# Weights laid out by partitions, x copied out of PSUM by ScalarE, another order in the tail of local attention, and the second channel weights a stage sooner

## The reference

```python
# 1: local attention, 8 heads of 64: |i - j| < 16 from the tokens themselves,
#    and 24 summaries of 32 tokens each (max of k, mean of v)
k_sum, v_sum = k.reshape(B,H,24,32,D).max(3), v.reshape(B,H,24,32,D).mean(3)
a = softmax([where(|i-j|<16, q k^T/8, -1e9), q k_sum^T/8 + log(32)]);  x = a @ [v; v_sum]
# 2: four experts, each a causal attention of one head of 64, two of four by a gate
logits = x @ w_gate;  w = softmax over the two largest
for e in range(4):
    out += w[e] * (softmax(causal((x @ wq[e]) (x @ wk[e])^T / 8)) @ (x @ wv[e])) @ wo[e]
# 3: mixing over tokens, then over channels
u = x + (relu(x^T @ w_tok1) @ w_tok2)^T
return u + relu(u @ w_ch1) @ w_ch2
```

## Time and profile before

| | us |
|---|---|
| median of 3 runs | 454.16 (452.81 to 454.59) |
| the profiled execution | 454.81 |
| its span, first to last instruction | 453.0 |
| PE busy | 432.1 (95%) |
| DVE busy | 300.1 (66%) |
| ACT busy | 219.9 (49%) |
| POOL busy | 150.6 (33%) |

### The profile page before, as it was taken

One profiled execution on the slowest core, in us unless ns is written; L12 is line 12 of the kernel. 1 busy time (PEld: TensorE's weight loads), 2 busy tenths in 40 slices (PEclk: granted clock), 3 DMA queues, 4 the chain that ended last, 5 costly groups with the idle time before them and its releaser, 6 DMA issues.

```text
span 453.0 us, 8596 instructions
## 1 busy us (share of the span) xinstructions
PE 432.1 (95%) x3332; PEld 365.7 (81%) x3332; DVE 300.1 (66%) x549; ACT 219.9 (49%) x579; POOL 150.6 (33%) x182
## 2 busy tenths in 40 slices
PE   8778998999997999999999989999999999999997
PEld 3557996787775789978887888998998898889885
DVE  4775379877567834697764977577675776465453
ACT  5856467655138946576682453344443233333120
POOL 3779382132116412002369436631232013100000
PEclk9989999999999999999999999999999999999999
DMA  8976137000393140000014111231133063201103
GB/s 244 227 200 182 36 101 283 1 2 0 112 299 97 25 140 2 0 1 1 0 49 140 46 48 30 65 93 48 46 95 93 0 234 93 61 33 48 46 2 139
DMA packets 16233, 38.11 MB, mean 84 GB/s; under 512 B 2064, under 2 KB 5312, under 8 KB 16192
## 3 DMA queue, kind: packets, MB, share of 16 engines
q1 hardware_dynamic: 15328, 35.98, 26.6%
q10 hardware_dynamic: 864, 1.57, 1.0%
HBM read 31.99 MB, written 4.72 MB: 81 GB/s over the span
## 4 chain that ended last, share of the span: by engine, by line
PE 83%; DVE 9%; issue 4%; ACT 3%; POOL 0%; DVEq 0%; POOLq 0%
PE ps_s L692 34%; PE ps_o L692 18%; PE ps_x L692 14%; PE ps_t L692 9%; PE ps_t L864 4%; PE ps_t L759 2%; ACT PA L1104 2%; DVE nmaxM L1440 1%; DVE nmaxA L1348 1%; PE ps_x L878 1%; DVE US L1502 1%; DVE PTA L1368 1%; DVE XT_l L1375 1%; DVE QS L1388 0%; DVE W_l L1526 0%
## 5 line engine op out<-in xcount | busy, mean ns | idle before, releaser
L1328 ACT ACTIVATE HID_h<-HID_raw 128x384 fp32r<-128x384 f32 x48 | 25.1, 525 | 73.2 <-DVE HID_raw L1656 33.0
L609 POOL TENSOR_TENSOR US<-X_h,X_l 128x512 f32<-128x512 f32 x12 | 15.4, 1280 | 86.0 <-DVE X_l L1479 55.2
L642 POOL TENSOR_TENSOR W_raw<-W_raw 128x256 f32<-128x256 f32 x11 | 11.4, 1041 | 92.4 <-DMA W_raw<-in_ch 92.4
L1104 ACT ACTIVATE PA<-ps_s,biasA 128x120 f32<-128x120 f32 x96 | 33.8, 383 | 14.7 <-DVE biasA L1352 14.7
L692 PE MATMUL ps_s<-C_h,HID_l 128*128 128x512 f32 x96 | 37.8, 393 | 0.0
L692 PE MATMUL ps_s<-C_l,HID_h 128*128 128x512 f32 x96 | 37.7, 393 | 0.0
L692 PE MATMUL ps_s<-C_h,HID_h 128*128 128x512 f32 x96 | 37.6, 392 | 0.0
L1645 DVE SCALAR_TENSOR_TENSOR HID_l<-HID_raw,HID_h 128x384 fp32r<-128x384 f32 x48 | 28.0, 587 | 10.8 <-ACT HID_h L1328 8.5
L550 POOL TENSOR_TENSOR PA<-PA,denA 128x480 f32<-128x480 f32 x24 | 23.7, 987 | 31.5 <-DVE denA L1361 31.4
L1167 ACT ACTIVATE PM<-ps_s,nmaxM 128x128 f32<-128x128 f32 (+5 forms) x48 | 30.1, 634 | 7.0 <-DVE nmaxM L1440 6.6
L692 PE MATMUL ps_o<-V_h,W_h 128*128 128x384 f32 x96 | 32.8, 342 | 0.1
(11 more groups left out here) (253 smaller groups left out, 1284.8 us busy)
## 6 DMA issues: line engine op xcount, KB each, us to landing
W_raw<-in_ch SPq DMA_DIRECT2D x12, 512.0 KB, 3.5
C_raw<-in_ch SPq DMA_DIRECT2D x12, 512.0 KB, 3.9
VW<-in_vw SPq DMA_DIRECT2D x12, 384.0 KB, 9.7
KP<-in_kT SPq DMA_DIRECT2D x8, 384.0 KB, 6.1
VT<-in_vT SPq DMA_DIRECT2D x8, 384.0 KB, 7.2
out_x<-US SPq DMA_DIRECT2D x12, 256.0 KB, 2.0
QT<-in_qT SPq DMA_DIRECT2D x7, 384.0 KB, 7.7
raw<-in_tok SPq DMA_DIRECT2D x4, 384.0 KB, 3.1
```

Source lines behind the costliest of these rows:

```text
L609: pool.tensor_tensor(US1[t][:, :], X2_h[:, t, :].bitcast(F32), X2_l[:, t, :].bitcast(F32), ALU.add).then_inc(m_xn, 1)
L642: pool.tensor_tensor(W[S3], W[A11], W[A21], ALU.subtract).then_inc(w_sum, 1)
L1104: last = act.activation(PA[:, u % NPA, j, :], ps_s[u % 2][:, j % 2, (j // 2) * KC:(j // 2 + 1) * KC], ACT.Exp, bias=biasA[:, u % 4, j:j + ...
L1328: act.activation(*own(s, n, half), ACT.Relu).then_inc(g_hi, 1)
```

## The change

Six things are done at once. The weights are laid out in DRAM by partitions, so that a chunk is one run for each partition, and w_gate becomes the last four columns of wv. For query tiles 0 to 4 ACT copies ps_x to US1, and the high and low part are then taken from US1; for tile 5 ACT copies after the low part; POOL's sum goes, and PE waits for the copy (m_xn) where it waited for the low part before it wrote ps_x. In the tail of local attention the transposes stand ahead of m_value(0), and m_value(2) behind the values of unit 9. SP loads the second set of channel weights right behind the first, DVE does second_row_sums ahead of the low part of tile 5, and POOL waits for two row_lows before it goes on with row sums. Scores 1 and 2 of batch 1 and its first means stand one token2 tile sooner.

```diff
-SCORES_BEFORE = (2, 4, 6)
-MEANS_BEFORE = 5
+SCORES_BEFORE = (2, 3, 5)
+MEANS_BEFORE = 4
...
             def load_weights(n):
-                (srcs, hi, _, cut) = chunks[n]
+                (src, hi, _, cut) = chunks[n]
                 if n >= 2:
                     sp.wait_ge(c_lo, n - 1)
-                for src, col in srcs:
-                    v = src.rearrange("(k p) n -> p k n", p=P)[:, cut[0]:cut[1], :]
-                    nk = cut[1] - cut[0]
-                    dst = raw[:, n % 2, 0:nk * hi.shape[-1]].rearrange("p (k n) -> p k n", k=nk)
-                    sp.dma_start(dst[:, :, col:col + v.shape[2]], v).then_inc(w_raw[n % 2], 16)
+                width = hi.shape[-1]
+                sp.dma_start(raw[:, n % 2, 0:(cut[1] - cut[0]) * width],
+                             src[:, cut[0] * width:cut[1] * width]).then_inc(w_raw[n % 2], 16)
...
             sp.wait_ge(m_s, B * MU)
             load_rows(0)
+            load_rows(1)
             sp.wait_ge(m_av, B * NVG)
-            load_rows(1)
             load_second(0)
             load_second(1)
...
-            def sum_x2(b, t):
-                pool.wait_ge(m_xl, b * TQ + (t + 1))
-                if b > 0:
-                    pool.wait_ge(st_u[t], b * 16)
-                pool.tensor_tensor(US1[t][:, :], X2_h[:, t, :].bitcast(F32), X2_l[:, t, :].bitcast(F32),
-                                   ALU.add).then_inc(m_xn, 1)
...
                 for t in range(TQ):
-                    sum_x2(b, t)
                     if b < B - 1 and t < 3:
                         key_windows(b + 1, 0, t)
...
+            pool.wait_ge(w_lo, 2)
             for s in range(2, STEPS):
                 row_sums(s)
...
-                    pe.wait_ge(m_xl, b * TQ + PROJECTED_BEFORE[t])
+                    pe.wait_ge(m_xn, b * TQ + PROJECTED_BEFORE[t])
...
-                    pe.wait_ge(m_xl, b * TQ + t)
+                    pe.wait_ge(m_xn, b * TQ + t)
...
                 if t < 2:
                     pe.wait_ge(m_hl, b * KT + (m + 1))
+                    pe.wait_ge(m_xn, b * TQ + TQ)
...
+                    if k <= NU + 2:
+                        a_transpose(b, k - 3)
                     if k == NU:
                         m_value(b, 0)
-                    if k == NU + 1:
-                        m_value(b, 2)
-                    if k <= NU + 2:
-                        a_transpose(b, k - 3)
                     if k >= 4:
                         a_values(b, k - 4)
-                    if k == NU:
-                        m_value(b, 1)
+                    if NU <= k <= NU + 1:
+                        m_value(b, k - NU + 1)
                     if k > NU:
                         m_project(b, k - NU - 1)
...
+            def m_x2_raw(b, t):
+                if b > 0:
+                    act.wait_ge(st_u[t], b * 16)
+                act.activation(US1[t][:, :], ps_x[:, :], ACT.Copy).then_inc(m_xn, 1)
+
             def m_x2(b, t):
+
                 act.wait_ge(m_wo, b * TQ + (t + 1))
-                act.activation(X2_h[:, t, :], ps_x[:, :], ACT.Copy).then_inc(m_xh, 1)
+                if t < TQ - 1:
+                    m_x2_raw(b, t)
+                    act.wait_ge(m_xn, b * TQ + (t + 1))
+                    act.activation(X2_h[:, t, :], US1[t][:, :], ACT.Copy).then_inc(m_xh, 1)
+                else:
+                    act.activation(X2_h[:, t, :], ps_x[:, :], ACT.Copy).then_inc(m_xh, 1)
+                    act.wait_ge(m_xl, b * TQ + TQ)
+                    m_x2_raw(b, t)
...
-                dve.tensor_tensor(X2_l[:, t, :], ps_x[:, :], X2_h[:, t, :].bitcast(F32),
-                                  ALU.subtract).then_inc(m_xl, 1)
+                dve.tensor_tensor(X2_l[:, t, :], US1[t][:, :] if t < TQ - 1 else ps_x[:, :],
+                                  X2_h[:, t, :].bitcast(F32), ALU.subtract).then_inc(m_xl, 1)
...
                 m_out_lo(b, TQ - 1)
+                if not more:
+                    second_row_sums()
                 m_x2_lo(b, TQ - 1)
                 for m in range(KT):
...
-                if not more:
-                    second_row_sums()
...
+    by_rows = lambda w: np.asarray(w).reshape(-1, P, np.asarray(w).shape[-1]).transpose(1, 0, 2).reshape(P, -1)
+    values = np.concatenate([columns(inputs["moe_wv"]), np.asarray(inputs["moe_w_gate"])], axis=1)
```

More of the change, by code:

```diff
@@ L361, in windows @@
             return bass.AP(tensor=rows.tensor, offset=rows.offset, ap=[rows.ap[0], [HALF, 4], [1, WK]])
-        chunks = [(((wv_d, 0), (wg_d, E * HD)), wv_h, wv_l, (0, KD)),
-                  (((wq_d, 0),), wq_h, wq_l, (0, KD)), (((wk_d, 0),), wk_h, wk_l, (0, KD)),
-                  (((wo_d, 0),), wo_h, wo_l, (0, EP))]
-        chunks += [(((tok1_d, 0),), tok1_h, tok1_l, (a, a + 3)) for a in (0, 3)]
-        chunks += [(((tok2_d, 0),), tok2_h, tok2_l, (a, a + 1)) for a in range(KT)]
+        chunks = [(wv_d, wv_h, wv_l, (0, KD)), (wq_d, wq_h, wq_l, (0, KD)), (wk_d, wk_h, wk_l, (0, KD)),
+                  (wo_d, wo_h, wo_l, (0, EP))]
+        chunks += [(tok1_d, tok1_h, tok1_l, (a, a + 3)) for a in (0, 3)]
+        chunks += [(tok2_d, tok2_h, tok2_l, (a, a + 1)) for a in range(KT)]
         N_WV, N_WQ, N_WK, N_WO, N_TOK1, N_TOK2 = 1, 2, 3, 4, 6, 8
@@ L536, in split @@
             def split(n):
-                srcs, hi, lo, cut = chunks[n]
-                landed[n % 2] += 16 * len(srcs)
+                _, hi, lo, cut = chunks[n]
+                landed[n % 2] += 16
                 pool.wait_ge(w_raw[n % 2], landed[n % 2])
@@ L553, in split_step @@
             def split_step(n, i):
-                (srcs, hi, lo, _) = chunks[n]
+                (_, hi, lo, _) = chunks[n]
                 src = raw[:, n % 2, 0:KD * hi.shape[-1]].rearrange("p (k n) -> p k n", k=KD)
                 if i == 0:
-                    landed[n % 2] += 16 * len(srcs)
+                    landed[n % 2] += 16
                     pool.wait_ge(w_raw[n % 2], landed[n % 2])
@@ L955, in turns @@
                         pe.wait_ge(m_ds, b * TQ + sum(SPREAD_AT[t] < k for t in range(TQ)))
-                        pe.wait_ge(m_xl, b * TQ + sum(TURN_AT[t] + 1 < k for t in range(TQ - 1)))
+                        pe.wait_ge(m_xn, b * TQ + sum(TURN_AT[t] + 1 < k for t in range(TQ - 1)))
                     c_transpose(0, j, turn_bank[x])
@@ L1704 @@
         "vT": by_pair(v).reshape(B, P, PAIRS * S),
-        "wq": columns(inputs["moe_wq"]), "wk": columns(inputs["moe_wk"]), "wv": columns(inputs["moe_wv"]),
-        "wg": inputs["moe_w_gate"], "wo": np.asarray(inputs["moe_wo"]).reshape(E * HD, DM),
-        "tok1": inputs["moe2_w_tok1"], "tok2": inputs["moe2_w_tok2"],
+        "wq": by_rows(columns(inputs["moe_wq"])), "wk": by_rows(columns(inputs["moe_wk"])), "wv": by_rows(values),
+        "wo": by_rows(np.asarray(inputs["moe_wo"]).reshape(E * HD, DM)),
+        "tok1": by_rows(inputs["moe2_w_tok1"]), "tok2": by_rows(inputs["moe2_w_tok2"]),
         "ch1": rows, "ch2": second,
```

2 lines of the change are left out of this document (1 added, 1 removed).

## The result

The changed kernel took 451.3 us (median of 5 runs, 451.07 to 452.24), the kernel before 454.16 (5 runs beside them, 452.81 to 454.63): a ratio of 0.9947 with a 95% interval of 0.9926 to 0.9968. The forecast was 453.8, its range 451.0 to 456.0. Run again later among the experiments, the changed kernel stood at 0.9981 [0.9956, 1.0006], an interval that takes in no change at all, so that the size is known only roughly: a gain of some 0.2 to 0.5%, about 1 to 2.5 us.

A forecast was written before the change was run, and what follows sets the result against it. PE was taken as the bound, nearly full except in local attention and before the channel stage; terms -1.3 + 0 + 0.5 + 0.4 + 0 = -0.4 gave 454.4 us as a profile, 453.8 as a median, range 451.0 to 456.0.

The forecast's parts named there:

- (a): Head of the channel stage: DVE's four sums get through between POOL's, -1.1 there, 452.3 us in total; chance 0.25.
- (b): As (a), with x copies fully hidden and the stop at 21.21 gone: -3.5, 450.7 us; chance 0.11.
- Where to look: From 262 us PE is busy 187.5 of 191 us; edits reach that part only by starting it earlier.
- 1, tail of local attention: Transposes ahead of m_value(0) let m_value(1) start 0.65 us sooner in each batch: -1.3 us, bounds -1.6 and -0.9.
- 2, layout: Weight loads at the start: value 0; -1.1 if the 21.21 stop goes, +0.6 if POOL's splits hit DVE's gate operations differently.
- Rival (d): Tail of local attention: the new order does nothing, the PTA copy replacing XT_l; total +0.9, 455.1 us; chance 0.08.
- no stop over 0.3 us before m_value(0): Sign of a right forecast: in either batch PE has no longer stop there in the tail of local attention.
- 3, x by ACT: Copies delay X_h and X_l by 0.65 us, showing at tile 3 of each batch: +0.5 us, working bound +1.5.
- 4, head of the channel stage: Wait for U goes (-1.1), but DVE and POOL take turns, delaying tile 5's X_l (+1.5): +0.4, bounds -1.1 and +0.8.
- over 1 us behind the end of X_h: Sign of a right forecast: X_l of tile 5 comes that late, at the head of the channel stage.
- 5, scores sooner: Start of batch 1: scores ready 2 us sooner, but ACT's queue holds unit 2's exponentials: 0, bounds -0.4 and +0.3.
- Rival (c): Slower through ACT's queue: 5 of 10 x copies pass on their 0.65 us delay; total +2.4, 456.6 us; chance 0.11.

The follow-up runs named there:

- e12: The changed kernel run once more, nothing altered: 450.92 us, ratio to the kernel before 0.9981 [0.9956, 1.0006].
- e6: The whole change without the weights' new layout: 452.04 us, ratio to the kernel before 0.997 [0.9948, 0.9991].
- e9: The changed kernel with batch 1's unit 2 exponentials ahead of ACT's last store and DVE's fourth second row sum behind tile 5's X_l: 449.38 us, ratio to before 0.9941.
- e11: As e9, but with the weights laid out as in the kernel before: 449.26 us, ratio to the kernel before 0.9915 [0.9883, 0.9947].
- e1: The kernel before with the weights' new layout alone: 453.64 us, ratio 1.0025 [1.0006, 1.0043].
- e3: The kernel before with x copied out by ACT alone, POOL's sums removed: 452.41 us, ratio 1.0002 [0.9985, 1.0018].
- e5: The kernel before with scores 1, 2 and the means of the next batch one token tile sooner, alone: 454.14 us, ratio 1.0021 [1.0000, 1.0042].
- e8: The changed kernel with batch 1's unit 2 exponentials moved ahead of ACT's last store of U: 451.04 us, ratio to the kernel before 0.9953 [0.9932, 0.9975].
- e10: As e8, with POOL's last column sums and first row sums waiting for DVE's four second row sums: 449.21 us, ratio to before 0.993 [0.9907, 0.9952].

## Why the prediction was right, and where it wasn't

The time lay in the range, by 0.3 us, and 2.5 us on the fast side of the forecast of 453.8, between rivals (a) with 452.3 and (b) with 450.7. As a ratio the first measurement is 0.53% faster, just over the bound of 0.5%, the second 0.19%, within it. The direction was right for a small gain; that the sum came as near as it did was in part luck. The single terms fared less well against the ledger: parts 2 and 5, taken as nothing, lost some 0.6 to 1.2 us between them, and parts 3 and 4, forecast to lose 0.9, won about 0.6.

**Where to look.** Right: nothing changed behind 266 us but the start of it.

**1, tail of local attention: -1.3, measured -1.32** (-0.65 and -0.67). The timeline of PE in the changed kernel, which answers to the earlier trace rows:

```profile
36.69 0.62 PE L750 MATMUL ps_t<-ident,PA 128*120 128x128 f32 x4 [0.91 <-DVE PTA L1371]
37.07 0.37 PE L683 MATMUL ps_s<-wv_h,XT_h 128*128 128x260 f32 x1
...
38.68 0.73 PE L683 MATMUL ps_o<-PTA,VW 120*64 120x64 f32 x16
39.35 0.39 PE L683 MATMUL ps_s<-wv_h,XT_h 128*128 128x260 f32 x1
```

The wait is for the PTA copy as the working has it, 0.91 instead of 1.28, and from there on nothing stops PE; the second value product follows the values of unit 8 at once. Rival (d) is out. The prediction's sign of being right, no stop over 0.3 us before m_value(0), contradicts its own working, in which PE stands from 38.05 (39.33 less 1.28) to 38.9, and it didn't come true.

**2, layout: 0, measured +0.3 to +0.9 in the trace** (e12 against e6, e9 against e11, e1 against before; more where the clock fell), and 1.0025 [1.0006, 1.0043] alone. This term failed in its value. Its upper bound, +0.6, was for just this, splits that fall onto the gate's operations in another way, but it was too low for two of the three pairs. I took the middle because I saw no PE wait on POOL, and the wait comes by way of DVE and ACT. In company the times don't show it (e6 against the changed kernel, e11 against e9). The whole stretch stands at +0.5 to +0.9 in the changed kernels without a drop, as some 0.2 of it is there with the old layout too, once the other parts are in (e6, e11). The lower bound, the "issue" stop at 21.21 freed, didn't come true: the stop is 2.2 us in the first profile of the changed kernel, and 0.85 in e3 and e5 with the old layout as in e8 with the new.

**3, x by ACT: +0.5, measured about -0.4.** The loss at tile 3 of batch 0 is there (+0.42, I had 0.2 to 0.3), but not where I put it. These rows are of before, and then of the changed kernel:

```profile
107.48 0.87 PE L864 MATMUL ps_t<-ident,PM 128*128 128x128 f32 x6
```

```profile
104.38 0.69 DVE L1482 TENSOR_TENSOR X_l<-US,X_h 128x512 fp32r<-128x512 f32 x1 [1.01 <-ACT X_h L1195]
...
106.64 0.84 PE L855 MATMUL ps_t<-ident,PM 128*128 128x128 f32 x6 [0.69 <-issue]
...
108.43 0.85 PE L855 MATMUL ps_t<-ident,PM 128*128 128x128 f32 x6 [0.17 <-issue]
109.64 0.50 PE L683 MATMUL ps_x<-wo_h,OT_h 128*128 128x512 f32 x1 [0.36 <-DVE OT_l L1477]
```

The new stop of 0.69 us is at the transposes one group sooner (107.48 before, without a stop). In front of them DVE has X_l, 0.7 us later than it was, then the score maxima, from 104.99, and ACT the exps PM, from 105.98, whose result these transposes read. The stop that I had counted on, 0.52 at 109.65, shrinks to 0.17, since it's the same delay taken earlier, and the one for OT_l goes from 0.30 to 0.36: 0.69 - 0.35 + 0.06 = 0.40. DVE's idle 0.45 ahead of OX, from which I worked, lies behind the place; the idle time ahead of X_l was 0.26 (before, at 105.06). Batch 1 keeps nothing of it (experts1 -0.06). What the step missed is the gain: I wrote that no wait on PE's path hangs on POOL's sums. But the OT_l of 1.13 us at 241.82, which I used as evidence in part 4, was stretched by one of them. In e3 it takes 0.57:

```profile
238.87 0.57 DVE L1480 TENSOR_TENSOR OT_l<-OX,OT_h 128x256 fp32r<-128x256 f32 x1 [0.49 <-ACT OT_h L1184]
```

PE's products with OT_l start 0.22 us sooner by it. The first of DVE's second row sums goes from 0.73 to 0.42 in e3 too, and all that DVE does behind it is that much sooner. One piece of this is the wait for U, from 1.06 to 0.87. The other is a stop too short for the bracket, at the first product into ps_t:

```profile
253.64 1.28 DVE L1502 TENSOR_TENSOR US<-ps_t,US 128x512 f32<-128x512 f32 x2
...
254.38 0.50 PE L692 MATMUL ps_t<-H_h,tok_h 128*128 128x512 f32 x1
```

These are of before. The product may overwrite ps_t when the first of the two additions has read it; that ends at 254.33 us and PE starts at 254.38, where matmuls elsewhere follow each other at 0.23 us and here at 0.40 and then 0.34. In e3 PE doesn't stop there and gains 0.27. With 0.06 at the first low part of H, 0.22 + 0.06 + 0.27 + 0.2 make up the head column of e3, -0.78.

**4, head of the channel stage: +0.4, measured -0.22 in company, -0.40 alone.** The mechanism is right: DVE and POOL take turns, X_l is late, the wait for U goes. The size was off. I priced a turn at 0.42 + 0.73 = 1.15 us; the rows above show a pace of 0.88, so that the four end at 244.4 and cost 3.6 us instead of 4.3. X_l is late by 0.8 instead of 1.5; the sign "over 1 us behind the end of X_h" is 0.78 for that reason. Rival (a), the four get through in 2.1 us, is wrong as a mechanism, though the trace's -0.4 alone lies between it and my sum; e10 shows what it would have taken: POOL idle. And 0.2 us of the 1.06 for U were the x copies' to win, which leaves less for this part in company.

**5, scores sooner: 0, measured +0.33 in company and +0.61 alone.** The reason why nothing is won held: ACT's queue has the exponentials of unit 2 behind the last stores, and e8 wins 1.1 us by moving them. Two things cost where the term had nothing. "PE's work is the same" overlooked that its order isn't: one more change between scores and token2, 0.27 us. And the store's delay costs 0.07 at the stop for PA in company, 0.34 alone. In the earlier trace rows ACT stood idle 1.40 us ahead of them, until their bias; in the changed kernel's row it is 2.63, until DVE's last addition, which is now behind unit 2's maxima in DVE's list.

**Rival (c)**, slower through ACT's queue, is out: of the ten copies one costs PE time, 0.42 us.

**The sum.** With the ledger's terms: -1.32, +0.5 to +0.9 (the whole gate stretch), -0.36, -0.22, +0.33, which is -1.1 to -0.7 against the -0.4 forecast and against -0.9 to -2.4 by the two timed ratios (0.9981 and 0.9947 of 452 to 454 us). The first measurement was helped by runs of before that lay high: their median of 454.16 is 452.1 to 452.9 over 96 runs on three chips. I put the profile's 0.65 us above its median and took that median for granted. A kernel before of 452.1 to 452.9 and the ledger's terms give 451.0 to 452.2, and 451.3 was measured: most of the distance from the forecast lies in the time of before, not in the parts.

## What to carry to other kernels

An instruction whose row is longer than its like elsewhere is a gain waiting for whoever moves its neighbour away: price the removal of a POOL instruction by the DVE rows that lie beside it, not only by who waits for it. When the work of two engines is made to share a stretch, measure the pace of a pair in the trace, and move only as many as fit the idle time: here three sums and not four, 0.75 us (or hold the other engine back, which won the same). When scores are made ready sooner, the queue of the engine that consumes them has to be reordered with them; doing the first without the second cost 0.6 us (0.3 in company) and doing both won 0.8. And count the places where an engine changes from one kind of work to another, even when its work stays the same. When a delay is followed along a queue, start with the idle time directly ahead of the delayed instruction, not with the next gap behind it.

## What the runs showed of the hardware

A DVE and a POOL instruction of 0.42 and 0.73 us, alone, go at 0.88 us a pair when each waits for the other engine in turn, less than the sum of 1.15. Weights in runs of 4 KB instead of 1 KB, and 13,914 instead of 16,233 packets, brought no gain that stands out of the spread in a start in which the DMA engines are full, and sooner is not better: with POOL's cast some 0.4 us sooner against the gate's operations, these and what follows them take 6.92 to 7.71 us together instead of 6.73 to 6.85. And the first 37 us vary by 1.05 us in one and the same kernel (33.43 and 34.48 in the changed one), as much as all five parts of the change together are worth, and by 4.1 over all fourteen profiles (33.3 to 37.4), so that two single profiles can't be subtracted end from end.
